# Two expert layers moved behind the last pair's first layer in a fused attention and soft mixture-of-experts kernel

## The reference

```
kv  = einsum('bhsd,bhse->bhde', k, v)          # B=8, H=8, S=576, D=64
out = einsum('bhsd,bhde->bhse', q, kv)
x   = out / rms(out) * g_norm                  # -> 4608 tokens x 512
logits = x @ phi                               # 4608 x 32 slots (8 experts x 4 slots)
d = softmax(logits over tokens);  slot_input = d.T @ x        # 32 x 512
for e in range(8):
    h = relu(slot_input[e] @ w1[e])            # 4x512 @ 512x1024
    slot_out[e] = h @ w2[e]                    # 4x1024 @ 1024x512
c = softmax(logits over slots);  result = c @ slot_out        # 4608 x 512
```

## Time and profile before

| | us |
|---|---|
| median of 3 runs | 171.89 (171.84 to 172.47) |
| the profiled execution, its own time | 171.86 |
| its span, first to last instruction | 170.5 |
| PE busy | 146.9 (86% of the span) |
| DVE, ACT, POOL busy | 87.5, 88.8, 59.5 |
| SP's hardware DMA queue, packets' share of 16 engines | 97.7% |
| mean granted TensorE clock | 0.972 |

### The profile page before, as it was taken

How to read it: one execution, slowest core, us unless ns; L and a number is a source line. 1 busy time by engine, 2 the same in 40 slices (tenths; PEclk the granted TensorE clock), 3 DMA queues, 4 the chain that set the end, 5 groups by cost and what they waited for, 6 DMA issues and landing times.

```text
span 170.5 us, 3975 instructions
## 1 busy us (share of the span) xinstructions
PE 146.9 (86%) x1704; PEld 101.8 (60%) x1704; DVE 87.5 (51%) x187; ACT 88.8 (52%) x230; POOL 59.5 (35%) x73
## 2 busy tenths in 40 slices
PE   7789799899899899999988999899999489989200
PEld 3468678799679787888885673423358243454000
DVE  1122159683676564847366999427885037219300
ACT  3027687787966878769498870104131045218300
POOL 7000707677556477382646589000000004000000
PEclk9999999999999999999999999999999999999855
DMA  5999999999999999999999999999899999999996
GB/s 193 414 426 423 442 420 444 465 423 411 493 421 419 419 467 436 439 414 469 428 409 454 411 458 414 432 396 436 375 423 438 461 419 402 419 416 430 428 458 259
DMA packets 3843, 71.63 MB, mean 420 GB/s; under 512 B 778, under 2 KB 778, under 8 KB 913
## 3 DMA queue, kind: packets, MB, share of 16 engines
q1 hardware_dynamic: 3425, 71.20, 97.7%
q0 software_dynamic: 400, 0.18, 0.4%
HBM read 61.94 MB, written 9.44 MB: 419 GB/s over the span
## 4 chain that ended last, share of the span: by engine, by line
PE 49%; DMA 28%; ACT 11%; DVE 3%; SPq 2%; issue 1%
PE psum L93 49%; DMA arena<-in_w_dram 15%; DMA arena<-in_kv_dram 13%; ACT arena L93 3%; ACT bd L93 3%; ACT sq L93 2%; SPq L93 2%; ACT part L93 1%; DVE ms L93 1%; ACT r L93 1%; ACT d L93 1%; DVE logits L93 1%; DVE d L93 0%; DVE part L93 0%; DVE arena L93 0%
## 5 line engine op out<-in xcount | busy, mean ns | idle before, releaser
L93 PE MATMUL psum<-bd,arena 128*128 128x192 f32 (+1 forms) x320 | 54.6, 335 | 2.9 <-ACT bd L93 2.0
L93 PEld LDWEIGHTS psum<-bd,arena 128*128 128x128 f32 (+1 forms) x320 | 45.2, 179 | 8.4 <-ACT bd L93 2.9
L93 PE MATMUL psum<-arena 128*64 128x64 f32 (+2 forms) x896 | 37.1, 270 | 4.4 <-DMA arena<-in_w_dram 2.5
L93 PEld LDWEIGHTS psum<-arena 128*64 128x64 f32 (+2 forms) x896 | 28.3, 129 | 16.4 <-issue 6.6
L93 DVE TENSOR_REDUCE ms<-sq 128x16 f32<-128x1024 f32 (+1 forms) x19 | 22.1, 1163 | 26.3 <-ACT sq L93 25.8
L93 POOL TENSOR_TENSOR arena<-arena,r 128x512 f32<-128x512 f32 x34 | 34.8, 1044 | 0.0
L93 POOL TENSOR_TENSOR part<-part,r 128x512 f32<-128x512 f32 x17 | 17.8, 1049 | 47.5 <-DVE r L93 47.5
L93 ACT COPY arena<-psum 128x512 f32<-128x512 f32 (+2 forms) x48 | 30.7, 649 | 6.1 <-PE psum L93 6.0
L93 ACT ACTIVATE sq<-psum 128x512 f32<-128x512 f32 x36 | 21.5, 597 | 9.6 <-PE psum L93 9.1
L93 ACT COPY part<-psum 128x256 f32<-128x256 f32 (+1 forms) x38 | 13.6, 359 | 12.5 <-DVE part L93 11.3
L93 DVE TENSOR_REDUCE logits<-part 128x64 f32<-128x512 f32 (+1 forms) x18 | 17.9, 992 | 0.1
(11 more groups left out here) (77 smaller groups left out, 108.4 us busy)
## 6 DMA issues: line engine op xcount, KB each, us to landing
arena<-in_w_dram SPq DMA_DIRECT2D x2, 8064.0 KB, 30.4
arena<-in_t_dram SPq DMA_DIRECT2D x1, 6912.0 KB, 37.9
arena<-in_w_dram SPq DMA_DIRECT2D x1, 6400.0 KB, 23.0
arena<-in_w_dram SPq DMA_DIRECT2D x3, 2048.0 KB, 19.3
arena<-in_kv_dram SPq DMA_DIRECT2D x2, 2304.0 KB, 23.4
arena<-in_kv_dram SPq DMA_DIRECT2D x1, 4608.0 KB, 42.8
arena<-in_w_dram SPq DMA_DIRECT2D x1, 4096.0 KB, 26.0
arena<-in_kv_dram SPq DMA_DIRECT2D x1, 3584.0 KB, 32.3
```

Of the source, the lines that this page charges most:

```text
L93: self.inst, self.token = method(*args, **kwargs), None
```

## The change

Two calls, `expert_y(0, 1)` and `expert_y(1, 1)`, the second half's layers of experts 0 and 1, leave their place between `combine(2)` and `pair_h(3)` and stand behind `expert_y(3, 0)`. Nothing else is changed.

```
@@ -1129,11 +1129,11 @@
     pair_h(2)
     load_w(6, [h_read[2]])
     combine(2)
-    expert_y(0, 1)
-    expert_y(1, 1)
     pair_h(3)
     expert_y(2, 0)
     expert_y(3, 0)
+    expert_y(0, 1)
+    expert_y(1, 1)
     for e in range(4, NE):
         y_made = expert_y(e, 0)
     chunks = [(k, f) for k in range(NCH) for f in range(2)]
```

## The result

| | kernel before | changed kernel |
|---|---|---|
| median, 20 executions each | 172.49 us | 171.83 us |
| lowest and highest | 171.66 to 172.85 | 171.62 to 172.15 |
| ratio | | 0.9972, 95% interval 0.9959 to 0.9984 |
| profiled execution, its own time (span) | 171.86 (170.5) | 171.93 (170.6) |

The time of the changed kernel is the one that was forecast, 171.9. But it is faster than the kernel before, by 0.28% (the ratio of the mean times, 172.31 and 171.83 us; the medians differ by 0.66 us, 0.38%), and the interval does not reach 1, where I had forecast no change: the median of before is not the 171.89 of the first three runs. Its 20 times form two groups, 13 from 172.25 to 172.85 and 7 from 171.66 to 172.00, and the change keeps only the lower one. The two profiled executions do not differ by that, since that of before belongs to the lower group.

The account below looks back on a forecast made before the run. The DMA byte stream was taken as the bound, with PE waiting for loads 2 and 4. Moved work fits before load 4 lands, so 0.0 us is added to the 171.89 median: 171.9 us, range 171.3 to 172.7.

Parts of the forecast that it names:

- The posts: Landings of load 2 (124.86 us) and load 4 (134.61 us) that PE must await; both hold, new waits 1.4 and 0.53 us.
- the 96 records: PE's matmul records between `pair_h(3)` and load 4's landing, 64 before: 5.87 us taken, range 5.2 to 6.4.
- the sum of 0.0 us: PE passes load 4's landing at 134.72 as before, so the whole change costs nothing; chance 0.86.
- the one on the clock: Slower rival: the clock halves in the new wait before `pair_h(3)`, ending 2.7 us late, 174.6, or 173.3 with queue cover; chance 0.02.
- the *new* wait of 1.4 us: PE idle between `pair_h(2)`'s end at 123.48 and load 2's landing at 124.86, opened by moving the layers.
- a stream that gets faster: Faster rival: calmer PE at 123.5 to 124.9 speeds loads 3 to 6; 0.4 us, 170.9 at best; chance 0.05.
- the last three: The prediction's closing chances: 0.06 faster, 0.87 no measurable change, 0.07 slower.
- the two slower rivals: PE late at `expert_y(6, 0)` behind load 4 (172.2 to 173.5; chance 0.05), and the clock falling in the new wait (0.02).
- the unseen: Something not seen, of either sign, no place or size given; chance 0.02, half counted as faster.
- my sum for a delay: A PE delay at 134.72 loses 0.20 us at the wait for load 6 and some 1.3 in the last store's queue.
- the start-up of a store: Part of the last store's 10.9 us to landing, estimated at 2.5 us, leaving some 1.3 us to hide a delay.

Follow-up runs that it names:

- lo_fill_late: Kernel before without `expert_y(0, 1)` and `expert_y(1, 1)`, with 8 matmuls of zeros in PE's wait for load 4: 171.80 us, ratio 0.9987.
- before_again: The kernel before run again unchanged: 8 of 12 executions with a low clock at 172.23 to 173.41 us, 4 others at 171.69 to 171.93.
- fill_gap: Kernel before in its own order, with 8 matmuls of zeros in PE's wait for load 4: 171.81 us, ratio 0.9985.
- left_out: Kernel before without `expert_y(0, 1)` and `expert_y(1, 1)` at all, the second half's sum starting at expert 2: 172.30 us.
- lo_fill_early: Kernel before without `expert_y(0, 1)` and `expert_y(1, 1)`, with 6 matmuls of zeros in PE's wait for load 2: 172.34 us, ratio 1.0000.
- wait_doubled: Kernel before without the first half's layers of experts 2 and 3, which lengthened the wait for load 4 to 2.91 us: 172.56 us.

## Why the prediction was wrong

**What held.** The posts: PE waits for load 2 for 1.50 us (1.4 predicted) and for load 4 for 0.85 (0.53 predicted; the 96 records took 5.39 us and not the 5.87 that I took, inside the 5.2 to 6.4 stated). Load 6 landed at 149.51 (149.29 predicted) and the last store was issued at 159.75 (159.5), in an execution that ran 0.4 us late from 111 us on. The clock stayed at 1.00 until 160. In an execution in which the clock does not fall, the sum of 0.0 us is right: 171.81 to 171.84 for before in three comparisons, 171.83 and 171.75 for the changed kernel, each a median. That the sum started from the right number was luck: of the 20 times of before 13 lie in the upper group, and of the three that I had, two and the profiled one lay in the lower.

**What failed.** The step is the one on the clock. I asked only whether the *new* wait of 1.4 us could let it fall, and dismissed that with a row: 2.3 us of idle at 1.00. The answer for the new wait was right (lo_fill_late, 0 of 12). But the row was of one execution, and in four to seven of ten executions of before the clock falls behind that very wait, so the old wait had a price that the change takes away. That rival, "the old wait sometimes costs the clock, and the change makes it short", gives faster by the share of low executions times 0.7 to 0.9 us: with 13 of 20 by their times, the nearest I have for the first comparison, 0.5 us or 0.3%, and the mean times differ by 0.49 us. It had no chance of its own in the text; the 0.06 for faster went to a stream that gets faster, which nothing shows. (The shares given don't quite add up to the last three either: the two slower rivals and half of the unseen make 0.08 and not 0.07.)

There was a sign. Of the three times of before one was 172.47, 0.6 us above the others, and I used it only to widen the range. That the profiled execution lay at 171.86, with the lower two, should have made me say which of two kinds of execution it shows.

**The mis-sized cover.** Had the clock been priced, my sum for a delay would still have been off: I put 1.3 us of a delay into the queue of stores and called the start-up of a store 2.5 us. The queue hid 0.5, and the last store, issued 1.2 to 1.4 us later, still took 10.4 us. With 1.3 the price of a fallen clock would have come out near zero.

**Still open.** Why a given execution falls and another does not, at the same wait, no run shows. Some low executions have a mean clock of 0.943 to 0.958, about two to almost four times as far below the usual 0.972 as the traced one (0.964). They are slower too: 15 of the 51 low executions of before are such, with a median of 172.86 us, against 172.47 for the other 36. More than one fall in an execution would fit that, or a longer one, but none of them was traced.

## What to carry to other kernels

A wait of the matmul engine that ends with a DMA is not free because the DMA would have come no sooner: what runs behind it may run at half the clock, and in only some of the executions, so that one trace can show the harmless kind. When the times of the kernel before spread by more than its interval, look for two groups and for the clock of each before pricing a change from one profile. Moving independent matmuls into the longest wait, or eight matmuls of zeros where there are none, cost nothing here and removed the upper group; splitting the wait in two was enough. Eighteen of them, which run past the landing, cost as much as the fall (0.84 us).

## What the runs showed of the hardware that I had not expected

The granted clock can be 1.00 all through a wait of 2.3 us and be at 1.2 GHz for the work behind it: in before_again it was 1.00 from 132.4 to 134.7 and 0.52 from 134.7 to 138.1, when PE was busy all the time. The wait itself never shows the fall. In the three low executions that were traced the matmuls resume at 134.68 (before_again), 134.87 (lo_fill_early) and 134.82 (wait_doubled), and in stretches of 0.2 us the clock is still 1.00 in the one in which they resume, and 0.50 from 135.0, 135.4 and 135.2 on. The price is paid by the 32 records after the wait (3.57 us for 1.93), not in it. And about 1.9 us of matmuls of zeros, whose result nobody reads, did as well as real work: 0 of 11 and 0 of 12 low executions with them (fill_gap, lo_fill_late), against 8 of 12 and 7 of 12 in the two kernels that differ from these by them alone (before_again, left_out).
